# Zero products on TensorE in the first pair's waits, a second tile of row maxima ahead of the norms on VectorE, and the local shares copied by ScalarE

## What is computed

```python
scores = where(causal, -1e9, q @ k.T / sqrt(D)); scores -= scores.max(-1)
a = exp(scores); a /= a.sum(-1) + 1e-9
local = a @ v
q_p = where(q > 0, q, exp(q) - 1) + 1
mem_out = (q_p @ M_prev) / (q_p @ z_prev + 1e-6)
g = 1 / (1 + exp(-beta))                      # one number a head
x = g * mem_out + (1 - g) * local             # 2304 tokens x 512
x = (silu(x @ w_gate) * (x @ w_val)) @ w_out
h = x @ w_in; out = where(h >= 1, h, where(h <= -1, 0, (h + 1)**2 / 4)) @ w_out2
```

## Time and profile before

| what | value |
|---|---|
| median of three runs | 984.82 us |
| the profiled execution | 984.26 us |
| its span, first to last instruction | 982.5 us |
| TensorE busy | 962.7 us, 98% |
| VectorE busy | 705.3 us, 72% |
| ScalarE busy | 462.8 us, 47% |
| GpSimd busy | 307.1 us, 31% |

### The profile page before, as it was taken

How to read it: one execution, slowest core, us unless ns; L and a number is a source line. 1 busy time by engine, 2 the same in 40 slices (tenths; PEclk the granted TensorE clock), 3 DMA queues, 4 the chain that set the end, 5 groups by cost and what they waited for, 6 DMA issues and landing times.

```text
span 982.5 us, 18781 instructions
## 1 busy us (share of the span) xinstructions
PE 962.7 (98%) x6328; PEld 921.0 (94%) x6328; DVE 705.3 (72%) x1370; ACT 462.8 (47%) x938; POOL 307.1 (31%) x291
## 2 busy tenths in 40 slices
PE   6999999999999999999999999999999999999998
PEld 4777777899999999999999999999999999999998
DVE  5888999577777555557555568888886777867766
ACT  5899999555445222324222246545543334433331
POOL 5677776166672000100000156576310010000000
PEclk9999999999999999999999999999999999999999
DMA  6545443379878755555555535667875744548321
GB/s 236 163 155 165 153 163 109 122 277 350 310 264 337 268 193 195 212 220 216 223 211 193 196 110 205 241 241 244 304 265 192 286 169 186 189 165 299 137 107 65
DMA packets 46156, 204.72 MB, mean 208 GB/s; under 512 B 5488, under 2 KB 5872, under 8 KB 46064
## 3 DMA queue, kind: packets, MB, share of 16 engines
q1 hardware_dynamic: 45920, 203.52, 57.0%
q10 hardware_dynamic: 144, 0.00, 0.0%
HBM read 147.33 MB, written 56.17 MB: 207 GB/s over the span
## 4 chain that ended last, share of the span: by engine, by line
PE 84%; ACT 5%; DMA 4%; DVE 3%; issue 3%; POOL 0%; SPq 0%; ACTq 0%; DVEq 0%; POOLq 0%
PE ps L1437 24%; PE ps L1439 24%; PE ps L1438 24%; PE ps L1412 5%; PE ps L1355 4%; ACT pt L809 3%; PE ps L1385 3%; DMA kept_ul<-wu_l 2%; DMA rbc<-rsums 1%; ACT rown L788 1%; DVE hid_l L1198 1%; ACT tmp L914 0%; DMA qk<-qk_in 0%; DMA wu_r<-w_up 0%; DVE negs L1043 0%
## 5 line engine op out<-in xcount | busy, mean ns | idle before, releaser
L1437 PE MATMUL ps<-xt_h,wu_h 128*128 128x384 f32 x840 | 281.7, 335 | 1.8 <-DVE hb L1181 0.9
L1439 PE MATMUL ps<-xt_h,wu_l 128*128 128x384 f32 x840 | 281.1, 335 | 0.0
L1438 PE MATMUL ps<-xt_l,wu_h 128*128 128x384 f32 x840 | 281.1, 335 | 0.0
L1437 PE MATMUL ps<-hid_h,wd_h 128*128 128x384 f32 x672 | 225.7, 336 | 2.4 <-DVE xy L1220 1.6
L1439 PE MATMUL ps<-hid_h,wd_l 128*128 128x384 f32 x672 | 224.9, 335 | 0.0
L1438 PE MATMUL ps<-hid_l,wd_h 128*128 128x384 f32 x672 | 224.9, 335 | 0.0
L1220 DVE TENSOR_TENSOR xy<-xy,ps 128x384 f32<-128x384 f32 x288 | 158.6, 551 | 70.0 <-PE ps L1439 69.1
L899 ACT ACTIVATE hid_h<-hid_r 128x768 fp32r<-128x768 f32 x84 | 70.8, 842 | 200.8 <-DVE hid_r L1194 139.8
L1437 PEld LDWEIGHTS ps<-xt_h,wu_h 128*128 128x128 f32 x840 | 157.8, 188 | 4.0 <-issue 3.0
L1438 PEld LDWEIGHTS ps<-xt_l,wu_h 128*128 128x128 f32 x840 | 157.8, 188 | 0.0
L1439 PEld LDWEIGHTS ps<-xt_h,wu_l 128*128 128x128 f32 x840 | 157.8, 188 | 0.0
(11 more groups left out here) (84 smaller groups left out, 1273.8 us busy)
## 6 DMA issues: line engine op xcount, KB each, us to landing
wu_l<-kept_ul SPq DMA_DIRECT2D x40, 896.0 KB, 7.5
wu_h<-kept_uh SPq DMA_DIRECT2D x40, 896.0 KB, 5.0
kept_uh<-wu_h SPq DMA_DIRECT2D x20, 896.0 KB, 6.4
kept_ul<-wu_l SPq DMA_DIRECT2D x20, 896.0 KB, 8.8
wd_h<-kept_dh SPq DMA_DIRECT2D x28, 512.0 KB, 3.7
wd_l<-kept_dl SPq DMA_DIRECT2D x28, 512.0 KB, 4.7
wu_r<-w_up SPq DMA_DIRECT2D x20, 512.0 KB, 4.6
qk<-qk_in SPq DMA_DIRECT2D x15, 640.0 KB, 5.1
```

Of the source, the lines that this page charges most:

```text
L1437: nc.tensor.matmul(dst, w_hi, v_hi, start=start, stop=False, skip_group_check=onto)
L1438: nc.tensor.matmul(dst, w_hi, v_lo, start=False, stop=False, skip_group_check=onto)
L1439: return nc.tensor.matmul(dst, w_lo, v_hi, start=False, stop=stop, skip_group_check=onto)
```

## The change

Three edits, all of the first pair. TensorE multiplies a block of `pt` that VectorE has set to zero, into a PSUM bank that nothing uses then: ten times ahead of all else, four times after `scores(0)`, eight times before `turn(0)`. VectorE sets that block first of all; it takes `tile_max(0)` ahead of the shares, and `tile_max(1)` between `phi(0)` and `norm_q(0)`. Two of the three writes of `cf` go to ScalarE, between `exp_q(1)` and `exp_tile(1)`.

```diff
@@ scalar, in the loop over pairs
                     exp_q(p + 1)
+                if p == 0:
+                    act.wait_ge(gone_set, 1)
+                    rest = gone[:].rearrange("p (h o) -> p h o", o=1)
+                    nc.scalar.activation(cf[:, :, 1:NT], rest.broadcast_to([P, 2 * NPAIR, NT - 1]), ACT.Copy).then_inc(cf_set, 1)
+                    nc.scalar.activation(cf[D:P, :, 0], gone[D:P], ACT.Copy).then_inc(cf_set, 1)
@@ vector
+            nc.vector.memset(pt[:, PTS - 1, 0], 0.0).then_inc(blank_set, 1)
             dve.wait_ge(consts, 1)
...
+            dve.wait_ge(maskf_set, 2)
+            tile_max(0)
             nc.vector.memset(cf[0:D, :, 0], 1.0).then_inc(cf_set, 1)
             nc.vector.reciprocal(gone[:], gexp[:, 1]).then_inc(gone_set, 1)
-            dve.wait_ge(gone_set, 1)
-            rest = gone[:].rearrange("p (h o) -> p h o", o=1)
-            nc.vector.tensor_copy(cf[:, :, 1:NT], rest.broadcast_to([P, 2 * NPAIR, NT - 1])).then_inc(cf_set, 1)
-            nc.vector.tensor_copy(cf[D:P, :, 0], gone[D:P]).then_inc(cf_set, 1)
-            dve.wait_ge(maskf_set, 2)
-            tile_max(0)
             phi(0)
+            tile_max(1)
@@ vector, in the loop over pairs
                     for k in range(1, SLOTS):
-                        tile_max(j + k)
+                        if p > 0 or k > 1:
+                            tile_max(j + k)
@@ tensor
+            def idle_products(n):
+                pe.wait_ge(blank_set, 1)
+                for _ in range(n):
+                    nc.tensor.matmul(ps[:, 6, 0:P], pt[:, PTS - 1, 0], pt[:, PTS - 1, 0], start=True, stop=True)
+            idle_products(10)
             pe.wait_ge(consts, 2)
@@ tensor, in the loop over pairs
+                if p == 0:
+                    idle_products(4)
                 if p < NPAIR:
                     scores_f(p)
...
                         scores(SLOTS * p + k)
+                    if p == 0:
+                        idle_products(8)
                     turn(SLOTS * p, (0, 1))
```

More of the change, by code:

```diff
@@ L158, in attention_two_ffns @@
         ld_dn = [sem(f"ld_dn{s}") for s in range(3)]
-        consts, masks, maskf_set = sem("consts"), sem("masks"), sem("maskf_set")
+        consts, masks, maskf_set, blank_set = sem("consts"), sem("masks"), sem("maskf_set"), sem("blank_set")
         gexp_e, gexp_1, gone_set, cf_set, gt_set = (
```

## The result

The changed kernel took 983.28 us (median of 20 runs, 982.2 to 985.16), the kernel before 984.91 (20 runs, 983.73 to 985.86): 1.63 us less, ratio 0.9984 with a 95% interval of 0.9977 to 0.999. That is a real gain, and within the 0.2% that were called no change. The forecast was 983.7.

What follows compares the result with a forecast made beforehand. With TensorE 98% busy, it took the first pair's waiting chain in the first twenty microseconds as the target: -0.34 (order) - 0.8 (clock) = -1.14 us, giving 983.7. Forecast's range 983.4 to 984.5; 8 in 10, 982.6 to 985.0.

Steps and rivals of the forecast that it cites:

- The clock, s: Shift of the end of the first pair's scores(0) from an earlier TensorE clock rise: -0.8 us, range 0 to -1.1.
- rival of unhidden loads: Weight loads do not hide behind products, so zero products outlast TensorE's waits: 986.4 to 988.4 us; chance 0.05.
- clock late: Clock does not rise in time, s = 0, tile_max(1) pushes norm_q to 13.42: +0.7, 985.5 us; chance 0.10.
- The memset and the reciprocal on the path: First pair, VectorE: both now stand between tile_max(0) and phi(0), adding 0.50 us to the path.
- if the norms wait for tile_max(1): Sign in the first pair's changed profile that would show the forecast wrong; tile_max(1) was expected before norm_q, in z's wait.
- the cover: VectorE's wait of 1.66 for GpSimd's product with z, said to hold tile_max(1)'s 1.09 wholly.
- The second tile's maxima: First pair: tile_max(1) ahead of norm_q takes 1.09 from behind it; transposes shrink the copy's gain from 0.59 to 0.34.
- mem_scale(3): First pair, VectorE: its 0.96 beside GpSimd's work was expected to stay, no gain counted.
- the case of 0.3 more: If mem_scale(3) slipped in front, GpSimd's v_scale would bound instead of VectorE's next-pair maxima, for 0.3 more.
- ScalarE: First pair: the two copies, at most 0.45 each, cost ScalarE nothing; leaving VectorE, they save nothing.
- What passes on: From the first pair to the end: a microsecond saved there is one saved at the end, if nothing later holds it.
- nothing passes on: A wait in a later pair or at the handover to the nets takes the gain: 984.8 us; chance 0.07.

Runs made afterwards that it cites:

- products-alone run: Kernel before plus only the zero products and their memset, VectorE and ScalarE in the old order; 985.05 against 985.01 us, ratio 1.0001.
- ten-only run: Changed kernel with only the ten first zero products, without the four and the eight; 983.27 against 984.36 us for the kernel before, ratio 0.999.
- order-alone run: Changed kernel without any zero products, keeping VectorE's new order and the copies on ScalarE; 985.69 against 985.01 us for the kernel before, ratio 1.0008.
- run with the maxima moved back: Changed kernel with the second tile's maxima, tile_max(1), behind the norms again; 984.10 against 985.01 us for the kernel before, ratio 0.999.
- repeated run: Changed kernel measured once more, nothing altered; 983.50 against 984.99 us for the kernel before, ratio 0.9986.
- run with the first, too early wait: Changed kernel with GpSimd's second-net subtractions waiting for VectorE's halves of the step before; 985.98 against 985.01 us for the kernel before, ratio 1.001.

## Why the prediction came out right

The time lay in the range and near the point, and the main mechanism was the one forecast, but two of its terms had the wrong size: the gain was 1.63 by the medians, not 1.14. The first pair gave 0.65 more than forecast, and the nets took a part of it back.

*The clock, s.* Forecast -0.8; the first scores ended at 7.16 for 7.96, which is -0.80. The products started at 1.03, one cost 0.427 cold (20 records, 4.64 with the tail) and 0.223 warm (16 records at 0.112); both lie in the forecast bounds. The rise came within the first scores, at 6.06. That the clock is what the products move is shown by the products-alone run and by the ten-only run. The rival of unhidden loads is excluded by the price of a product; the rival "clock late" did not occur, but its mechanism did in the order-alone run. There the medians are 0.68 over before, about the 0.7 that I gave it, but in the profiled execution it cost 2.4: I had let only the scores run cold, and not the transposes and the next pair's scores.

*The memset and the reciprocal on the path.* Forecast +0.50. They overlapped, and phi(0) started 0.27 after the maxima ended (8.68 to 8.95). The product with z was done at 11.28 for it, not at 11.55. tile_max(1) ended at 11.41, just where the forecast's terms put it (12.21 - 0.80), but now after the product with z, and the norms followed it. That is the sign named ahead, "if the norms wait for tile_max(1)": the maxima did not lie wholly beside the product, the cover was short by 0.13, and the memset and the reciprocal were not on the path, as the run with the shares behind phi(0) shows. It made the norms earlier and not later, 11.41 against 11.59 by the forecast's terms.

*The second tile's maxima.* The copy shifted from 16.04 to 14.68, by -1.36; forecast -1.14.

*mem_scale(3).* This is the term that failed: "it comes against the same GpSimd work again, so I count no gain for it." It took 0.23 and not 0.96, since VectorE reached it at 16.44, before GpSimd's long product at 16.61. It moved by -1.86 and the product by -1.35: it waits for ScalarE's last exponentials, and ScalarE, which had taken the second tile's early, was done with them 1.86 sooner. Then GpSimd's v_scale bounded the second pair's values (TensorE waited 0.16 for it, 19.63), which I had named as the case of 0.3 more. It was worth 0.43. Together with the 0.22 above, the first pair gave 1.79 instead of 1.14. That this term hangs on who comes first is shown by the run with the maxima moved back.

*ScalarE.* Right: the copies took 0.29 and 0.26 beside VectorE's maxima. The forecast had leaving VectorE save nothing against before; in the new order, where the shares stand behind the maxima, it saves 0.57.

*What passes on.* "A microsecond saved there is a microsecond of the end" held for the pairs and in part for the nets. The rival "nothing passes on" had a share: 1.2 of the 1.8 in the profiled execution, and little in the medians (1.63 of the first trace's 1.79; 1.49 of the 1.54 in the repeated run). The 1.06 near 664 and 680 us is the contention of GpSimd and VectorE: the run with the subtraction in two halves takes it away. The 0.16 at the start of the nets is what is left of a longer wait of TensorE at 204 us (0.60 before, 1.65 changed), after two later ones of 0.21 and 0.25 had gone. At 202 us ScalarE waits for a store of weights to land before it may overwrite them; whether that store holds TensorE there no run tested.

## What to carry to other kernels

Look for the parts of a change that pay only together: here a faster engine gained nothing while its reader stood in line behind other work, and the reader's new order gained nothing while the engine was slow. Where VectorE and GpSimd both read SBUF, their order can be set by hundredths of a microsecond, as it was here, and a shift upstream can turn it; shorten the instruction that blocks before you try to time it. And follow a small gain to the end of the program: the place at which it is lost may be 600 us away, and here mending it gave about as much again as the change itself.

## What the runs showed of the hardware

- Products of zeros with themselves count as work for TensorE's clock: after twenty records it rose from 1.2 to 2.4 GHz within the first scores (6.06 us), and not at 14.37.
- A wait of 1.75 us of TensorE between two bursts could be followed by the lower level (the ten-only run, granted clock 0.50 from 9 to 12 us), though the burst behind it had already begun. With products in the same waits, which left 0.65 and 0.47, the level stayed up (the transposes took 1.07).
- The clock can fall late in the program too. In the run with the first, too early wait TensorE waited 1.91 us at 204 us, and the stretch behind it reads:

```profile
204.00:210.00 6.00, 5.57 (x23) 5.60 (x24) 4.78 (x7) 3.28 (x6) 3.62 (x4) 0.72 0.78 282
```

  In the run with the subtraction in two halves TensorE waited 2.18 at the same place, longer, and its products kept starting every 0.17 us behind it, as at the higher level: the length of the wait alone does not tell whether the clock falls. Three of the changed kernel's 20 runs have a mean clock of 0.998 instead of 1.0; they took 984.12, 984.83 and 985.16, its three slowest.
- The granted clock's column reads 1.00 until the first rise, whatever the level is the earlier trace rows. There the durations of equal instructions tell it.
- A GpSimd subtraction of 128x768 cost 1.84 where it went first, and the first half of a split one, 128x384, 1.01. The second half always came behind VectorE (1.73); by an estimate from the first, the split costs GpSimd some 0.2 each time.
